# The last tile's scores put in place by TensorE, and a rearranged first routing, in a fused attention and two-mixture kernel

## The reference

```python
# 1 attention: a band of 31 positions around each query, and 24 block maxima of the keys / block means of the values
scores = where(|i - j| < 16, q @ k.T / 8, -1e9) ; scores_s = q @ max_of_32(k).T / 8 + log(32)
x = softmax([scores, scores_s]) @ [v, mean_of_32(v)]
# 2 mixture with a skip: only tokens with x @ w_skip > 0 are computed
e = argmax(x @ w_gate) ; x += softmax(x @ w_gate)[e] * (relu(x @ w1[e]) @ w2[e])
# 3 mixture with equal shares: the (token, expert) pairs are taken in falling order of score,
#   a pair counts if its token is free and its expert has fewer than 384 tokens
logits = x @ w_gate2 ; out[token] = relu(x @ w1[assigned]) @ w2[assigned]
```

## Time and profile before

| | us |
|---|---|
| median of 3 runs | 827.86 |
| lowest and highest run | 825.83, 828.58 |
| the profiled execution | 829.41 |
| its span, first to last instruction | 825.4 |

### The profile page before, as it was taken

How to read it: one execution, slowest core, us unless ns; L and a number is a source line. 1 busy time by engine, 2 the same in 40 slices (tenths; PEclk the granted TensorE clock), 3 DMA queues, 4 the chain that set the end, 5 groups by cost and what they waited for, 6 DMA issues and landing times.

```text
span 825.4 us, 13873 instructions
## 1 busy us (share of the span) xinstructions
PE 727.5 (88%) x4561; PEld 504.0 (61%) x4561; DVE 359.0 (43%) x1458; ACT 220.7 (27%) x685; POOL 192.3 (23%) x251
## 2 busy tenths in 40 slices
PE   3788998998299999997219999999999999999995
PEld 2788988998287678675115555455555545555552
DVE  3577786886411121122583726537273563600000
ACT  2677787884011111111001111110211111021210
POOL 8275645452111111111010020202102020211001
PEclk9799999999599999999557999999999999999998
DMA  9898987587691618800033521507043160642000
GB/s 212 188 207 201 224 205 173 134 213 238 223 382 35 232 32 322 315 8 3 6 126 119 191 90 50 220 13 255 25 166 109 33 243 14 254 174 105 30 0 38
DMA packets 130466, 119.88 MB, mean 145 GB/s; under 512 B 95858, under 2 KB 95858, under 8 KB 130224
## 3 DMA queue, kind: packets, MB, share of 16 engines
q1 hardware_dynamic: 118192, 88.45, 35.2%
q10 hardware_dynamic: 6464, 14.73, 5.9%
q0 software_dynamic: 5760, 16.03, 5.7%
HBM read 105.95 MB, written 16.50 MB: 148 GB/s over the span
## 4 chain that ended last, share of the span: by engine, by line
PE 78%; DVE 9%; issue 3%; SPq 3%; DMA 3%; POOL 1%; ACT 1%; ACTq 0%; POOLq 0%; DVEq 0%
PE bank L1121 21%; PE bank L1136 21%; PE bank L1017 9%; PE bank L1034 8%; PE bank L877 3%; PE bank L898 3%; PE bank L1062 2%; PE bank L920 2%; SPq L465 2%; PE bank L887 2%; PE bank L1094 1%; DVE scratch L1346 1%; DVE shared L1357 1%; PE bank L997 1%; PE bank L864 1%
## 5 line engine op out<-in xcount | busy, mean ns | idle before, releaser
L1121 PE MATMUL bank<-scratch,weights 128*128 128x384 f32 x512 | 177.4, 499 | 0.7 <-ACT scratch L1302 0.7
L1136 PE MATMUL bank<-weights,scratch 128*128 128x512 f32 x384 | 175.2, 600 | 0.0
L1121 PEld LDWEIGHTS bank<-scratch,weights 128*128 128x128 f32 x512 | 94.3, 192 | 64.3 <-issue 9.8
L1136 PEld LDWEIGHTS bank<-weights,scratch 128*128 128x128 f32 x384 | 69.6, 190 | 70.7 <-issue 68.4
L1205 ACT ACTIVATE scratch<-shared,neg_max 128x120 f32<-128x120 f32 x192 | 73.4, 383 | 33.0 <-DVE neg_max L1357 20.9
L1308 ACT ACTIVATE scratch<-bank 128x384 f32<-128x384 f32 x64 | 31.4, 491 | 152.8 <-PE bank L1121 152.8
L664 POOL TENSOR_TENSOR scratch<-scratch,row_inv 128x480 f32<-128x480 f32 x48 | 47.3, 986 | 78.7 <-DVE row_inv L1367 78.5
L1017 PEld LDWEIGHTS bank<-mix,weights 128*128 128x128 f32 x512 | 60.8, 197 | 5.2 <-issue 5.2
L1017 PE MATMUL bank<-mix,weights 128*128 128x128 f32 x512 | 61.7, 279 | 1.5 <-DVE mix L1571 1.5
L822 POOL DMA_INDIRECT out<-scratch,idx x24 | 25.2, 1049 | 147.4 <-ACT scratch L1314 145.6
L1034 PE MATMUL bank<-weights,mix 128*128 128x512 f32 x128 | 58.2, 597 | 0.0
(11 more groups left out here) (225 smaller groups left out, 941.6 us busy)
## 6 DMA issues: line engine op xcount, KB each, us to landing
weights<-in_moe_w SPq DMA_DIRECT2D x20, 2048.0 KB, 8.3
scratch<-in_moe_w SPq DMA_DIRECT2D x8, 2048.0 KB, 15.5
weights<-in_moe_w ACTq DMA_DIRECT2D x16, 512.0 KB, 6.1
mix<-in_v SPq DMA_DIRECT2D x40, 192.0 KB
rows<-row SPq DMA_DIRECT2D x24, 264.5 KB, 3.6
weights<-in_k SPq DMA_DIRECT2D x24, 256.0 KB, 5.2
scratch<-in_q SPq DMA_DIRECT2D x24, 256.0 KB, 4.4
weights<-in_v ACTq DMA_DIRECT2D x24, 192.0 KB, 4.1
```

The costliest lines, as they stand in the source:

```text
L1121: last = mm(hb2[f % 2][:, 0:CAP], w1_sb[odd][:, c, f * P:(f + 1) * P], xT2[odd][:, c, :], start=(c == 0), stop=(c == C - 1), skip_group_ch ...
L1136: last = mm(yb2[c % 2][:, :], hT2[odd][:, f, c * P:(c + 1) * P], w2_sb[odd][:, f, :], start=(f == 0), stop=(f == FC - 1), skip_group_check ...
```

## The change

Five things change.

1. The scores of the last tile no longer go through `rows`. SyncE reads the scores as soon as the scatter before the last has landed, and GpSimd's last scatter waits for that read. VectorE makes two one-hot factors from the last tile's list (`last_row`, `last_tile`) and the product `last_part`; PE turns them into a mask of the tokens of that tile and into their scores in place; VectorE clears these tokens in `scores2` and adds the scores.
2. `judge` runs for 20 tiles inside VectorE's attention loop (behind `copy_logits(20)`, `g` = 44) and for the last four behind it. PE's last `gates` stands ahead of its last `turn_rows`.
3. The numbers of tiles come from totals: VectorE adds up the choices of each partition, PE sums them over partitions between two of the `ranks` products, and VectorE rounds up with integer steps, without waiting for all of `ranks`.
4. `high_hot` and `ids_hot` are laid out in pairs of tiles, as `low_hot` is, and are made first; `low_hot` is made in two halves, each with its own signal to PE.
5. The first gather of the second mixture reads `token_list` directly, each of its thirds has its own semaphore, and PE turns a third when it is there. Some constants are set before the first mixture instead of behind it.

`judge` itself is as before; its definition has moved ahead of the loop.

```diff
+    TOTALS_AT = 8
+    JUDGED = 20
...
-        high_hot = part(SLOTS, NT, dt=BF16)
-        ids_hot = part(2, SLOTS, NT, dt=BF16)
+        high_hot = part(NT // 2, SLOTS, 2, dt=BF16)
+        ids_hot = part(2, NT // 2, SLOTS, 2, dt=BF16)
...
-        iota_slots = sb("iota_slots", [P, SLOTS, NT], BF16)
+        iota_slots = sb("iota_slots", [P, SLOTS, 2], BF16)
...
-            sp.wait_ge(s.scattered, 16 + 16 * (ends[E - 1] + 1))
+            sp.wait_ge(s.scattered, 16 + 16 * ends[E - 1])
             sp.dma_start(scores2, rows[:, 0:E].rearrange("(j p) e -> p j e", p=P)).then_inc(s.scores_in, 16)
...
+            pool.wait_ge(s.scores_in, 16)
             nc.gpsimd.tensor_copy(idx_out[:, :], slot_list[:, bass.ds(total, 1)]).then_inc(s.lists_in, 1)
             wait_apart(pool, s.lists_in, 2 * total + 1)
...
-            gather2(0, 0)
+            pool.wait_ge(s.token_list_made, 1)
+            for c in range(CT):
+                nc.gpsimd.indirect_dma_start(
+                    out=xg2[0][:, c, :], out_offset=None, in_=rows,
+                    in_offset=bass.IndirectOffsetOnAxis(ap=token_list[:, c:c + 1].bitcast(U32), axis=0),
+                    bounds_check=N - 1, oob_is_err=False).then_inc((s.first_rows0, s.first_rows1, s.first_rows2)[c], 16)
+            nc.gpsimd.tensor_copy(idx2[0][:, :], token_list[:, 0:CT]).then_inc(s.expert_list_in, 1)
+            pool.wait_ge(s.expert_list_in, 2)
...
+                if g == HT + 1:
+                    gates(NT - 1)
                 if g % 2 == 1 and g >= 3:
                     turn_rows((g - 3) // 2)
-            gates(NT - 1)
...
+                if j == TOTALS_AT:
+                    pe.wait_ge(s.chosen_sum, 1)
+                    mm(totals[:, 0:E], ones[:, :], chosen_n, start=True, stop=True, skip_group_check=True
+                       ).then_inc(s.totals_ps, 1)
             last.then_inc(s.ranked_ps, 1)
-            pe.wait_ge(s.phase_ready, 2)
             for j in range(NT):
+                if j % (NT // 2) == 0:
+                    pe.wait_ge(s.phase_ready, 2 + j // (NT // 2))
                 last = mm(table[:, 0:2 * SLOTS], low_hot[:, j // 2, :, j % 2],
-                          ids_hot[:, :, :, j].rearrange("p a b -> p (a b)"), start=(j == 0), stop=(j == NT - 1))
+                          ids_hot[:, :, j // 2, :, j % 2], start=(j == 0), stop=(j == NT - 1))
             last.then_inc(s.table_ps, 1)
...
+            pe.wait_ge(s.last_tokens, 1)
+            mm(bank[1][:, 256:256 + NT], last_row, last_tile, start=True, stop=True, skip_group_check=True
+               ).then_inc(s.last_ps, 1)
+            pe.wait_ge(s.last_scores, 1)
+            mm(bank[2][:, 0:NT * E], last_row, last_part.rearrange("p j e -> p (j e)"), start=True, stop=True,
+               skip_group_check=True).then_inc(s.last_ps, 1)
...
+            def turn2(i, par, first=False):
+
+                if first:
+                    pe.wait_ge(s.first_rows0, 16)
+                else:
+                    pe.wait_ge((s.gathered2_0, s.gathered2_1)[par], 16 * CT * ((i - par) // 2 + par))
                 for c in range(CT):
+                    if first and c:
+                        pe.wait_ge((s.first_rows0, s.first_rows1, s.first_rows2)[c], 16)
...
+                if g == 2 * JUDGED + 4:
+                    dve.wait_ge(s.consts_pool, CONSTS + 1)
+                    v_.memset(chosen_h[:, NT, :], 0.0)
+                    link(judge(0, JUDGED))
...
-                wide = [P, NT // 2, P, 2]
-                v_.tensor_tensor(out=low_hot,
...
-                wide = [P, SLOTS, NT]
-                link(v_.tensor_tensor(out=high_hot, in0=iota_slots[:, :, :],
...
+                wide = [P, NT // 2, SLOTS, 2]
+                link(v_.tensor_tensor(out=high_hot,
+                                      in0=iota_slots[:, :, :].rearrange("p (o n) s -> p o n s", o=1).to_broadcast(wide),
+                                      in1=hi_h.rearrange("p (j o s) -> p j o s", o=1, s=2).to_broadcast(wide),
+                                      op=ALU.is_equal))
+                v_.tensor_scalar(ids_hot[:, 0, :, :, :], high_hot, iota_p1[:, 0:1], None, ALU.mult)
+                v_.tensor_tensor(out=ids_hot[:, 1, :, :, :], in0=high_hot,
+                                 in1=iota_tile[:, :].rearrange("p (j o s) -> p j o s", o=1, s=2).to_broadcast(wide),
+                                 op=ALU.mult)
+                for a_, b_ in ((0, NT // 4), (NT // 4, NT // 2)):
+                    wide = [P, b_ - a_, P, 2]
+                    v_.tensor_tensor(out=low_hot[:, a_:b_, :, :],
+                                     in0=iota_pair[:, :, :].rearrange("p (o n) s -> p o n s", o=1).to_broadcast(wide),
+                                     in1=lo_h[:, 2 * a_:2 * b_].rearrange("p (j o s) -> p j o s", o=1, s=2
+                                                                          ).to_broadcast(wide),
+                                     op=ALU.is_equal).then_inc(s.phase_ready, 1)
...
-            dve.wait_ge(s.consts_pool, CONSTS + 1)
-            v_.memset(chosen_h[:, NT, :], 0.0)
-            link(judge(0, NT - 1))
             copy_logits(NT - 1)
-            judge(NT - 1, NT).then_inc(s.phase_ready, 1)
+            judge(JUDGED, NT).then_inc(s.phase_ready, 1)
+            dve.wait_ge(s.phase_ready, 1)
+            with nc.allow_low_precision(reason="whole numbers up to 24"):
+                v_.tensor_reduce(chosen_n, chosen_h[:, 0:NT, :].rearrange("p j e -> p e j"), AX, ALU.add
+                                 ).then_inc(s.chosen_sum, 1)
             copy_gates(NT - 1)
             v_.memset(tile_bounds[:, 0:1], 0)
-            dve.wait_ge(s.ranked_ps, 1)
...
-            count = ranks[:, NT * E:(NT + 1) * E]
-            link(v_.tensor_tensor(out=over, in0=count.rearrange("p (e o) -> p e o", o=1).to_broadcast([P, E, NT]),
-                                  in1=iota_128t[:, :].rearrange("p (o j) -> p o j", o=1).to_broadcast([P, E, NT]),
-                                  op=ALU.is_gt))
-            link(v_.tensor_reduce(tiles, over, AX, ALU.add))
+            dve.wait_ge(s.totals_ps, 1)
+            link(v_.tensor_scalar(tiles_i, bank[4][:, 0:E], float(P - 1), None, ALU.add))
+            link(v_.tensor_scalar(tiles_i, tiles_i, 7, None, ALU.arith_shift_right))
+            link(v_.tensor_copy(tiles, tiles_i))
             link(v_.tensor_scalar(tiles[:, 0:1], tiles[:, 0:1], 1.0, None, ALU.max))
             ends_f = base[0]
...
             link(v_.tensor_scalar(tiles, tiles, float(P), None, ALU.mult))
+            dve.wait_ge(s.ranked_ps, 1)
             link(v_.tensor_tensor(out=place, in0=ranks[:, 0:NT * E].rearrange("p (j e) -> p j e", e=E),
                                   in1=over_tokens(tiles), op=ALU.add))
...
+            for x, val in ((open_e, 1.0), (free_t, 1.0)):
+                v_.memset(x, val)
+            v_.memset(room_e, float(CAP))
+            v_.memset(reach, 0.0)
+            link(v_.memset(assigned, 0.0))
+            link(v_.tensor_scalar(first_digits[:, :], digit_row[:, :], SHIFTS[0], None, ALU.logical_shift_left))
+            half = ROUND_KEYS[0] // 2
+            v_.tensor_scalar(first_keys[:, 0:half], first_digits[:, 0:half], -1, None, ALU.bitwise_xor)
+            link(v_.tensor_scalar(first_keys[:, half:], first_digits[:, half:], -(1 << 31), None, ALU.bitwise_xor))
...
+            last_id = slot_list[:, bass.ds(total, 1)]
+            v_.tensor_scalar(last_lo_i, last_id, P - 1, None, ALU.bitwise_and)
+            link(v_.tensor_scalar(last_hi_i, last_id, 7, None, ALU.arith_shift_right))
+            v_.tensor_copy(last_lo, last_lo_i)
+            link(v_.tensor_copy(last_hi, last_hi_i))
+            v_.tensor_scalar(last_row, iota_row[:, :], last_lo, None, ALU.is_equal)
+            link(v_.tensor_scalar(last_tile, iota_t[:, :], last_hi, None, ALU.is_equal))
+            credit(dve, s.last_tokens)
+
             dve.wait_ge(s.logits2_done, CREDIT + total + 1)
+            v_.tensor_tensor(out=last_part, in0=over_experts(last_tile), in1=over_tokens(bank[0][:, 0:E]), op=ALU.mult
+                             ).then_inc(s.last_scores, 1)
             v_.tensor_scalar(xp[:, 0:E], bank[0][:, 0:E], 0.0, None, ALU.add).then_inc(s.row2_made, 1)
...
+            dve.wait_ge(s.last_ps, 1)
+            link(v_.tensor_scalar(others, bank[1][:, 256:256 + NT], -1.0, 1.0, ALU.mult, ALU.add))
             dve.wait_ge(s.scores_in, 16)
+            link(v_.tensor_tensor(out=scores2, in0=scores2, in1=over_experts(others), op=ALU.mult))
+            dve.wait_ge(s.last_ps, 2)
+            link(v_.scalar_tensor_tensor(out=scores2, in0=bank[2][:, 0:NT * E].rearrange("p (j e) -> p j e", e=E), scalar=0.0,
+                                         in1=scores2, op0=ALU.add, op1=ALU.add))
```

111 lines of the change are left out of this document (56 added, 55 removed).

## The result

| us | before | after |
|---|---|---|
| median (lowest to highest), 20 runs of each | 829.85 (825.83 to 834.19) | 824.05 (819.27 to 829.88) |
| the profiled execution, its span | 829.41, 825.4 | 825.51, 823.1 |

The ratio is 0.9927, 95% interval 0.9909 to 0.9945 (a ratio is estimated from all runs of a comparison, so it can differ from the quotient of two medians by up to 0.3%): faster by 5.8 us, not by 7.95, and 824.05 lies outside the predicted range of 817.3 to 823.2. The miss of 4.15 us has two parts: 2.0 us because the kernel before took 829.85 over 20 runs where the three known ones had 827.86, and 2.15 us of the effect itself.

The account below looks back on a forecast made before the run. PE sets the pace in both mixtures, so only the VectorE-PE chains leading to their first products could gain. First routing -1.85, scores -6.0 and thirds -0.1 made -7.95 us: from 827.86 to 819.9 us, range 817.3 to 823.2.

Parts of the forecast that it names:

- Part 1, the judging: End of attention: judging 20 tiles inside the loop makes the masking 1.8 us later and the ranks 0.7 us later.
- the fall of the clock: Rival: in attention PE's pause grows to 2.4 us, the clock halves until the ranks, +8.9, giving 828.8 us; 3%.
- Part 2, totals: First routing, first rank product to the place: starts at +2.6 instead of +3.25 us, -0.65 us.
- the bound named: Totals in the first routing: +0.2 us if PE is at its lower clock and the full ranks come last.
- Part 3, the list: First routing, wide comparison to table reading: 4.2 instead of 6.4 us, -2.2 us, with 57 ns a product.
- First gather: First gather of the first routing, issued while weight loads still fill the queues: +0.3 us (0 to +1.5).
- Part 4, the scores: Entry of the second routing: last tile's scores ready early, start at 391.0 instead of 397.01, -6.0 us.
- Part 5, thirds: First gather of the second mixture: PE can use only 0.2 us of what is saved, -0.1 us.
- The sum: Whole kernel: -1.85 - 6.0 - 0.1 = -7.95 us, from a base median of 827.86 to 819.9 us.

Follow-up runs that it names:

- the filled pause: The changed kernel with 18 more TensorE transposes of the identity in the pause that the judging leaves, run twice: 821.35 us, 0.9879, then 819.81, 0.989.
- the scores part alone: The kernel before with only the last tile's scores put in place by TensorE and the routing constants moved ahead: 822.29 us, ratio 0.9902.
- the judging alone: The kernel before with only the judging of tiles 0 to 19 moved into attention in one piece: 832.16 us against 830.46, ratio 1.0022.
- the changed kernel, last time: The changed kernel run again unedited, as the base of its batch: ratio 0.991 to the kernel before.
- the experiment: The changed kernel with all judging behind the loop and the list's one-hots in 48-byte steps again: 822.2 us, ratio 0.9903.
- all judging behind: The changed kernel with the judging of all 24 tiles back behind the attention loop, run twice: 820.8 us, 0.9872, then 817.68 us, 0.9881.

## Why the prediction was wrong, step by step

**Part 1, the judging: the step that failed.** The order of events was right: masking 1.9 us later (1.8), PE's wait over 2 us, and 0.72 us of delay (0.7), as the filled pause shows. What failed is the sentence that priced PE's pause by its length alone and gave the fall of the clock 3%. It rested on the window 202 to 204 in the earlier trace rows, which lies inside a pause of 2.7 us and shows 1.00. But the same trace has the clock down one microsecond after PE had resumed at 204.70, which the next windows would have told:

```profile
204.00:206.00 2.00, 1.30 (x21) 1.30 (x22) 0.70 (x7) 0.00 (x0) 0.00 (x0) 0.90 0.94 171
206.00:208.00 2.00, 0.26 (x9) 0.17 (x5) 1.49 (x8) 0.00 (x0) 0.00 (x0) 0.50 1.01 400
```

Nor does the clock always hold inside this pause. The kernel with the scores part alone has the same program up to here, and in its profile the clock fell at 202.3, 1.4 us into the same pause, which ends at 203.63:

```profile
202.00:204.00 2.00, 0.37 (x3) 0.35 (x4) 1.49 (x13) 0.00 (x0) 0.00 (x0) 0.57 1.10 300
```

After the change it fell in four profiles of four, and with the judging alone in the fifth. In PE's 7.4 us of attention work and what follows, that cost 1.6 to 4.9 us, 3.3 in the mean. So the rival named the mechanism; its price, 8.9 for a fall lasting until the ranks, was too high, and so the result lies between it and the forecast.

The Trainium skill ("TensorE: Matmul & The Clock Gate", Part 1) says that the number of slow products at a kernel's start differs between runs of one kernel. The traces show a spread of that kind behind a pause in the middle of a kernel: 10.2, 3.4, 6.8 and 6.8 us behind the same pause.

**Part 2, totals.** 3.08 us from ranks to places instead of 3.25, so -0.17, where -0.65 was forecast; PE was at half clock there, the bound named. But the 3.25 of the profile before were run at full clock for their first 0.9 us. Like against like the part gives more than forecast: at half clock all the way 3.08, where the old code took 4.06 (scores part alone), -0.98; at full clock (the changed kernel, last time) 2.42, at least -0.83.

**Part 3, the list.** 4.23 us from first comparison to table (4.2 forecast, 6.38 before). The step between the elements was the reason for 1.34 us of it, by the experiment: 72 ns a product, against 129. The 57 taken for it were too low. The Trainium skill ("SBUF — State Buffer", section "Door 1: The DMA port swizzle") has reads that stay within a line of 16 bytes at full speed, and others slower. The trace agrees in the direction, 72 ns with the 4-byte step against 129 with the 48-byte one.

**First gather.** From issue to PE's turn 4.61, 3.79, 3.87 and 4.23 us with the weight loads moved beside it, 3.75 and 3.74 with all judging behind, where the queues' share falls from 1.0 as the gather is issued: +0.4 (0.3 forecast). The 4.94 of the profile before was itself a long one (3.54 and 3.66 in the two other kernels with its list), so the comparison with it hides this. The prediction's reason, that most of those 4.9 us pass before the bytes move, was not right: the windows before show bytes from 220.0 to about 222, so 1.9 us pass ahead of them and some 1.1 behind.

**Part 4, the scores.** -6.17 (-6.0), and the read was issued 5.7 us ahead of the last gate scores' product. **Part 5, thirds.** -0.2 (-0.1).

**The sum.** With the measured terms: clock +3.3, judging +0.7, totals -0.2 to -0.8, list -2.15, gather +0.4, scores -6.2, thirds -0.2, makes -4.35 to -4.95; 5.8 were measured (4.6 to 7.6 by the interval). One term was missing from the sum, the half clock behind the pause, and the runs of one kernel lie 8 to 11 us apart, so the median of three was a base good to 2 us only.

## What to carry to other kernels

Before moving work into a stretch where TensorE is busy, ask how long it makes TensorE's longest pause, and look for the clock behind the pauses that the trace already has as well as inside them, in more than one profile: here a pause of 2.7 us showed 1.00 to its end in one profile and the fall in the middle of it in another. A long insertion on another engine is cheaper in pieces that lie in that engine's own waits; where it can't be cut, some useless products in the pause pay for themselves, if no instruction that others wait for, as a register load, is queued behind them.

## What was not expected of the hardware

- The clock falls behind shorter pauses too, but not always: four kernels have the same instructions up to the ranks, with 9 transposes ahead of them and, behind R, pauses of 0.58, 0.43 and 0.50 us; two kept 1.00 there, two fell, at 203.7 and 206.7; and the changed kernel, last time, kept it from 202.5 to 212.7 through a pause of 1.26. The pause makes the fall likely; these traces don't say what decides.
- One batch was slower in all its kernels, the one before too (835.78). There PE waited for VectorE's counts between the products of the second mixture, 5.5 to 6.9 us in 4 or 5 waits of up to 1.4; the changed kernel, the same program, doesn't wait there at all in the profiles of the other batches. The second mixture took 392 to 393 us, not 386. Why stays open.
